# Down products of two pairs in alternate steps, a convolution partly on TensorE at the head, and four places for h's square at the end

## The chip, the cores and the metric

The kernel runs on one core of a Trainium2 chip, as one program. The metric is the device time of one execution in microseconds. TensorE is called PE in the profile, VectorE DVE, ScalarE ACT, GpSimd POOL; SP only issues transfers. DMA queues are marked with a q (SPq, POOLq).

## The reference

Three parts follow one another on 8192 rows of 192 features. First a causal convolution of seven taps over the rows, per head of 24 features, with softmax weights. Then two feed-forward layers of width 2048.

```
w = softmax(weight)                                   # 8 heads x 7 taps
x = sum_k w[head, k] * x_padded[row + k, feature]     # 2 sequences of 4096 rows
h = x @ w_in ;  g = h / (1 + exp(-1.702 h)) ;  x = g @ w_out          # layer 1
h = x @ w_in2 ; P = a0 + a1 h + a2 h^2 + a3 h^3
Q = 1 + |b0| |h| + |b1| h^2 ;  g = P / (Q + 1e-6) ;  out = g @ w_out2 # layer 2
```

## The kernel before

**Tiles and steps.** The rows are worked in 16 tiles (`TILES`) of 512 (`NT`), with features on the partitions. The 192 features are a part a of 128 and a part b of 64. The 2048 columns of a layer are 16 units of 128, taken two at a time: such a pair of units of one tile is a duo in the code, a pair in this text. There are 8 per tile (`DUOS`) and 128 in all (`TOTAL`). The program of each engine is a loop over steps n = 8 i + s. In step n TensorE makes h of layer 1's pair n (`up`, `up_rest`), the down products of layer 1's pair n - 1, h of layer 2's pair n - 10 (`LAG_UP2`) and the down products of layer 2's pair n - 12 (`LAG_DOWN2`). Steps 0 to 9 have layer 1 alone, steps 128 to 139 layer 2 alone (`alone(n)`). Every engine has its own stream in program order; all order between engines is by semaphores that the code writes out by hand. A wait on one engine holds all that stands behind it there.

**Precision.** Each layer's up product is split in high and low parts (`x_a_hi`, `x_a_lo`, `up_a_lo`) in fp32r: eight products of 128 rows per pair and layer (lines `L329` to `L332`), and two of 64 rows (`L356`, `up_rest`), the latter of the two layers side by side on different row halves. Layer 1's 128 output columns are made from parts in fp32r too, six products per pair (`down_a_parts`, `L375` to `L377`), from `g_nhi` and `g_low`. The remaining down products are plain fp32, which the trace shows as two matmuls each: layer 2's 128 columns (`down_a`, `L362`) and both layers' 64 columns (`down_b`, `L382`; for the first tile `down_b_apart`, `L388`). Layer 1's 64 columns go to rows 64 to 127 of the bank `acc_b`, layer 2's to rows 0 to 63.

**The other engines in a step.** ScalarE: for layer 2 `t1` (`L598`), the square of h (`L609`, into `sq`, two places), its absolute value (`L611`); then layer 1's gelu (`L615`, into L1.g, two places) and its rounded negative (`L617`); then for the pair before in layer 2 `s1` and `s2` (`L638`, `L639`) and the reciprocal's seed (`L644`). VectorE: `t2`, `t3`, `q` (`L808`, `L810`, `L811`), `z2` and g (`L832`, `L836`), `z1` (`L846`), and operations of the next tile's convolution (`conv_ops`, `L739`, `L740`), placed by `CONV_AT` and, for tile 1, by `CONV_AT_FIRST`. The reciprocal's product m is GpSimd's (`L961`). From pair 10 on `g_low` comes by two transfers: SP copies g, and POOL's queue adds `g_nhi` to it (`L967`); for the first ten pairs VectorE makes it (`L849`).

**Between the layers.** At s = 0 (`S_X2`) of the next tile ScalarE (`x_a_hi`, `L625`) and VectorE (`L800` to `L802`, `L839`) read layer 1's sums as layer 2's x. At s = 3 (`S_ACC2`) ScalarE copies layer 2's sums into `y_b` and `y_a`; at s = 0 and 1 of the tile after, TensorE turns them and ScalarE writes `y_out`.

**The head.** TensorE turns tile 0 of x, VectorE convolves parts a and b (14 taps), ScalarE rounds the result and the weights' high parts, VectorE makes low parts. Five products with the unit matrix (`L533`) stand before the first step; they have no use in the result.

## Time and profile before

| what | value |
|---|---|
| median of 3 runs | 1317.26 us (1317.21 to 1319.43) |
| the profiled execution | 1320.08 us |
| its span on the core | 1318.3 us |
| TensorE busy, matmuls | 5072 |
| VectorE, ScalarE, GpSimd busy | 1126.2, 1093.1, 533.4 us |
| DMA moved | 148.60 MB, mean 113 GB/s |

The profile is of one execution; the span is what its engines cover, and the execution's time has some 2 us around it. A matmul's end in the records is modelled, so consecutive starts tell more than durations. The idle time before an instruction is printed in brackets with what ended it.

### The profile page before, as it was taken

The numbers are of one execution on the slowest core, as the hardware profiler recorded it, in microseconds if no ns is written. First come the engines' busy times: TensorE is split into PE (matmuls) and PEld (weight loads), VectorE is DVE, ScalarE is ACT, GpSimd is POOL, SyncE is SP. The second block draws the span as 40 slices with busy tenths as digits, with TensorE's granted clock in tenths as the row PEclk, the third lists the DMA queues.
The fourth block names the chain that finished last, engine by engine and source line by source line (L and its number), as shares of the span: only waits on it lengthen the run. The fifth ranks groups of instructions, "written<-read, shape, count | busy, mean of one in ns | idle before, by whom it ended". The sixth has DMA issues, their size and how long they took to land. (4 is left out here: it accounts for less than half of the span.)

```text
span 1318.3 us, 15217 instructions
## 1 busy us (share of the span) xinstructions
PE 1279.1 (97%) x5072; PEld 747.0 (57%) x5072; DVE 1126.2 (85%) x1233; ACT 1093.1 (83%) x1250; POOL 533.4 (40%) x383
## 2 busy tenths in 40 slices
PE   6999999999999999999999999999999999999786
PEld 3556556565665656556565665655556565565432
DVE  6668998989888898988989898898989889777886
ACT  6568898888888888888888888888888888888674
POOL 2414444344443444444444443444434444444221
PEclk9999999999999999999999999999999999999898
DMA  7234445545455554544545454454544555454000
GB/s 183 85 76 114 114 113 132 124 120 136 110 125 117 129 126 115 136 110 124 124 122 134 107 140 113 124 124 109 139 113 124 123 125 116 108 131 105 13 0 24
DMA packets 107822, 148.60 MB, mean 113 GB/s; under 512 B 20961, under 2 KB 45281, under 8 KB 107745
## 3 DMA queue, kind: packets, MB, share of 16 engines
q0 software_dynamic: 33984, 61.88, 27.5%
q1 hardware_dynamic: 73284, 85.75, 19.4%
q8 instruction: 40, 0.66, 0.2%
q14 instruction: 37, 0.30, 0.1%
q10 hardware_dynamic: 477, 0.01, 0.0%
HBM read 13.64 MB, written 6.29 MB: 15 GB/s over the span
## 5 line engine op out<-in xcount | busy, mean ns | idle before, releaser
L961 POOL TENSOR_TENSOR work<-work 128x1024 f32<-128x1024 f32 x127 | 305.1, 2402 | 538.2 <-ACT work L611 491.2
L967 POOL DMA_DIRECT2D g_low<-g_nhi x236 | 207.8, 1015 | 189.8 <-DMA g_low<-g 183.5
L382 PE MATMUL acc_b<-g,down 128*64 128x512 f32 x512 | 248.7, 608 | 11.5 <-DVE g L836 11.4
L362 PE MATMUL acc_a<-g,down 128*128 128x512 f32 x512 | 255.1, 621 | 0.0
L808 DVE TENSOR_TENSOR work<-work,h 128x1024 f32<-128x1024 f32 x128 | 156.3, 1221 | 112.3 <-ACT work L611 110.8
L382 PE MATMUL acc_b<-g,down_b 128*64 128x512 f32 x480 | 231.7, 605 | 0.0
L598 ACT ACTIVATE work<-h,par 128x1024 f32<-128x1024 f32 x128 | 142.5, 1113 | 97.7 <-PE h L356 93.2
L329 PE MATMUL h<-x_a_hi,up_a_hi 128*128 128x512 f32 x510 | 206.8, 406 | 11.1 <-DVE x_a_lo L839 5.5
L331 PE MATMUL h<-x_a_hi,up_a_lo 128*128 128x512 f32 x510 | 199.9, 392 | 0.0
L330 PE MATMUL h<-x_a_lo,up_a_hi 128*128 128x512 f32 x510 | 199.9, 392 | 0.0
L332 PE MATMUL h<-x_b,up_b_hi 128*128 128x512 f32 x510 | 199.6, 391 | 0.0
L638 ACT ACTIVATE work<-work 128x1024 f32<-128x1024 f32 x127 | 134.8, 1062 | 68.0 <-POOL work L961 68.0
L362 PEld LDWEIGHTS acc_a<-g,down 128*128 128x128 f32 x512 | 87.4, 190 | 166.4 <-issue 166.4
L810 DVE SCALAR_TENSOR_TENSOR work<-work,par,h 128x1024 f32<-128x1024 f32 x128 | 164.0, 1281 | 4.5
L811 DVE SCALAR_TENSOR_TENSOR work<-work 128x1024 f32<-128x1024 f32 x128 | 156.2, 1220 | 0.0
L836 DVE SCALAR_TENSOR_TENSOR g<-work 128x1024 f32<-128x1024 f32 x117 | 143.4, 1226 | 11.0 <-issue 0.5
L375 PE MATMUL acc_a<-g_nhi,down_nhi 128*128 128x512 f32 x256 | 150.0, 586 | 2.4 <-DVE g_low L849 1.7
L846 DVE SCALAR_TENSOR_TENSOR work<-work,par 128x1024 f32<-128x1024 f32 x117 | 149.7, 1279 | 1.1 <-ACT work L644 1.1
L615 ACT ACTIVATE g<-h 128x1024 f32<-128x1024 f32 x128 | 132.5, 1035 | 12.8 <-PE h L356 12.8
L832 DVE SCALAR_TENSOR_TENSOR work<-work 128x1024 f32<-128x1024 f32 x117 | 142.7, 1220 | 0.0
L617 ACT ACTIVATE g_nhi<-g 128x1024 fp32r<-128x1024 f32 x128 | 135.9, 1062 | 4.0
L382 PEld LDWEIGHTS acc_b<-g,down 128*64 128x64 f32 x512 | 59.8, 136 | 133.2 <-issue 119.5
(131 smaller groups left out, 1946.7 us busy)
## 6 DMA issues: line engine op xcount, KB each, us to landing
g_low<-g SPq DMA_DIRECT2D x236, 256.0 KB, 2.4
g_low<-g_nhi POOLq DMA_DIRECT2D x236, 256.0 KB, 3.8
out<-y_out SPq DMA_DIRECT2D x15, 384.0 KB, 3.0
x_in<-in_x SPq DMA_DIRECT2D x16, 256.0 KB, 3.1
x_in<-in_x SPq DMA_DIRECT2D x32, 64.0 KB, 2.7
work<-in_moe_w_in SPq DMA_DIRECT2D x8, 256.0 KB, 4.4
work<-in_moe_w_in SPq DMA_DIRECT2D x16, 128.0 KB, 4.6
x_b<-x_hb SPq DMA_DIRECT2D x30, 64.0 KB, 2.1
```

The source lines that it names most:

```text
L329: mm(h, l.up_a_hi[:, cols], l.x_a_hi[:, p, :], start=True, stop=False)
L330: mm(h, l.up_a_hi[:, cols], l.x_a_lo[:, p, :], start=False, stop=False)
L331: mm(h, l.up_a_lo[:, cols], l.x_a_hi[:, p, :], start=False, stop=False)
L332: mm(h, l.up_b_hi[:, cols], l.x_b[:, p, :], start=False, stop=False)
L362: done = mm(L2.acc_a[:], L2.down[:, f, 0:P], L2.g[:, slot, k, :], start=f == 0, stop=f == STEPS - 1)
L375: mm(acc, down_nhi[:, f, :], g_nhi[:, slot, k, :], start=f == 0, stop=False)
L382: return mm(acc_b[l.acc_row:l.acc_row + DB, :], l.down_b[:, f, :], l.g[:, slot, k, :], start=f == 0, stop=f == STEPS - 1)
L808: tt(tu, tu, h, ALU.mult).then_inc(t2_ready, 1)
L810: stt(tu, tu, par[:, 1:2], h, ALU.add, ALU.mult).then_inc(t3_ready, 1)
L811: stt(sk, ab, 1.0 + 1e-6, sk, ALU.add, ALU.add).then_inc(q_ready, 1)
L961: tt(m, sq[v % 2], seed, ALU.mult).then_inc(m_ready, 1)
L967: pool.dma_start(g_low[:, n % 2, k, :], g_nhi[:, n % 2, k, :], accum_op=ALU.add)\
```

## The change

Four things change.

1. **Down products.** Before, every step has the 64-column products of both layers and layer 2's 128-column ones. Now even steps have the 64-column products of two pairs (layer 1's n - 2 and n - 1, layer 2's n - 14 and n - 13), odd steps layer 2's 128-column products of two pairs (n - 13 and n - 12). Layer 1's products from parts stay in every step. `downs` becomes `downs_b` and `downs_a`, with lists `downs1_b`, `downs2_b`, `downs2_a`. The use of g is counted apart for the two kinds (`g1_b_used`, `g2_a_used`, `g2_b_used`), L2.g has three places, and gelu waits for both counts. `S_ACC2` moves from 3 to 4. VectorE's x2 copies move behind `z1`.
2. **The head.** Twelve products of the unit matrix with itself stand ahead of the transposes. ScalarE makes seven diagonal matrices of tap weights, and TensorE convolves part b of tile 0 with them into the bank `first_b`; VectorE does part a alone. Three fillers stay, each behind a tap (`WARM_AFTER`). x_b is rounded before x_a. Tile 1 of x is loaded and turned one step earlier, its convolution spread otherwise, the root's rounds move into steps 0 and 1, and layer 2's weights are made in steps 4 to 7.
3. **The last steps.** `sq_of` gives the square of h two more places, those of L1.g, from pair 122 on (pairs with k % 4 of 2 or 3), so that the square waits for g of four pairs back.
4. **The turn to the end.** In step 128 layer 2's second up product comes after the down products, and x2's low parts are made right behind `q`.

```diff
-S_XT_FIRST = (2, 3)
+S_XT_FIRST = (1, 2)
-S_ACC2 = 3
+S_ACC2 = 4
+S_ACC2_ALONE = 3
-S_WEIGHTS2 = (2, 3, 4, 5)
+S_WEIGHTS2 = (4, 5, 6, 7)
-WARM_AFTER = 9
+WARM_AFTER = (12, 14, 16)
-    CONV_AT_FIRST = (0, 0, 0, 3, 10, NX, NX, NX, NX)
+    CONV_AT_FIRST = (0, 0, 0, 9, 13, NX, NX, NX, NX)
...
+        L2.g = sb("g2", [P, 3, 2, NT])
...
+        def sq_of(k):
+            return L1.g[:, k % 2, :, :] if k + LAG_UP2 >= TOTAL + 2 and k % 4 >= 2 else sq[k % 2]
...
+        def downs2_a(n):
+            if n >= TOTAL + 2:
+                pairs = [n - LAG_DOWN2]
+            else:
+                pairs = [n - LAG_DOWN2 - 1, n - LAG_DOWN2] if n % 2 else []
+            return [v for v in pairs if live(v)]
+        def downs2_b(n):
+            if n == TOTAL + 2:
+                pairs = [n - LAG_DOWN2 - 2, n - LAG_DOWN2 - 1, n - LAG_DOWN2]
+            elif n > TOTAL + 2:
+                pairs = [n - LAG_DOWN2]
+            else:
+                pairs = [n - LAG_DOWN2 - 2, n - LAG_DOWN2 - 1] if n % 2 == 0 else []
+            return [v for v in pairs if live(v)]
+        def downs1_b(n):
+            return [v for v in (n - LAG_DOWN1 - 1, n - LAG_DOWN1) if live(v) and n % 2 == 0]
...
+                    for k in range(2):
+                        if live(v2):
+                            if last(v2):
+                                pe.wait_ge(last_g2, k + 1)
+                            done2 = down_b(L2, e2, v2 % 3, k)
+                        if live(v1):
+                            unit = down_b_apart if v1 < DUOS else down_b
+                            done1 = unit(L1, e1, v1 % 2, k)
...
-                if alone(n):
-                    if n == TOTAL:
-                        up_alone(n)
+                if n == TOTAL:
+                    up_alone(n)
+                elif alone(n):
                     up_alone(n + 1)
-                downs(i, s, v1, v2)
+                downs_b(n)
+                downs_a(n)
+                if n == TOTAL:
+                    up_alone(n + 1)
...
+            for _ in range(12):
+                mm(L1.acc_a[:, 0:P], ident[:], ident[:], start=True, stop=True)
             transpose_x(0, 0)
             transpose_x(0, 1)
             pe.wait_ge(x_evacuated, 2)
-            pe.wait_ge(conv_steps, WARM_AFTER)
-            for _ in range(5):
+            pe.wait_ge(conv_steps, 1)
+            for k in range(taps):
+                pe.wait_ge(diagonal_ready, k + 1)
+                done = mm(L2.h[:, 0, 0:HALF], diagonal[:, k, :], xt_b[:, k:k + HALF], start=k == 0, stop=k == taps - 1)
+            done.then_inc(first_b_done, 1)
+            for count in WARM_AFTER:
+                pe.wait_ge(conv_steps, count)
                 mm(L1.acc_a[:], ident[:], xt_a[:, HALO:], start=True, stop=True)
...
                     wait(act, g1_used, n - 1)
+                    wait(act, g1_b_used, n - 1)
                     fn(L1.g[:, n % 2, :, :], L1.h[:], ACT.Gelu_apprx_sigmoid).then_inc(g1_ready, 1)
```

TensorE, a steady step before, from its last 64-row product on:

```order
L356 MATMUL h2<-x_b2,up_b_lo 128x512
L382 MATMUL acc_b<-g2,down2 64x512 [waits g2_ready,g1_ready]
L382 MATMUL acc_b<-g1,down_b1 64x512
L382 MATMUL acc_b<-g2,down2 64x512
L382 MATMUL acc_b<-g1,down_b1 64x512
L362 MATMUL acc_a2<-g2,down2 128x512 x2
L375 MATMUL acc_a1<-g_nhi,down_nhi 128x512 [waits g1_low_0]
L376 MATMUL acc_a1<-g_nhi,down_nlo 128x512
L377 MATMUL acc_a1<-g_low,down_hi 128x512
```

TensorE now, an even step at the same place (down1's 64 columns are `down_b1`, `L415` is `down_b`, `L408` is `down_a_parts`):

```order
L389 MATMUL h2<-x_b2,up_b_lo 128x512
L415 MATMUL acc_b<-g2,down2 64x512 [waits g2_ready,g1_ready,x2_lo_done]
L415 MATMUL acc_b<-g1,down_b1 64x512
L415 MATMUL acc_b<-g2,down2 64x512
L415 MATMUL acc_b<-g1,down_b1 64x512
L415 MATMUL acc_b<-g2,down2 64x512 [waits g2_ready,g1_ready]
L415 MATMUL acc_b<-g1,down_b1 64x512
L415 MATMUL acc_b<-g2,down2 64x512
L415 MATMUL acc_b<-g1,down_b1 64x512
L408 MATMUL acc_a1<-g_nhi,down_nhi 128x512 [waits g1_low_2]
L409 MATMUL acc_a1<-g_nhi,down_nlo 128x512
```

TensorE now, an odd step at the same place (`L395` is `down_a`):

```order
L389 MATMUL h2<-x_b2,up_b_lo 128x512
L395 MATMUL acc_a2<-g2,down2 128x512 [waits g2_ready]
L395 MATMUL acc_a2<-g2,down2 128x512
L395 MATMUL acc_a2<-g2,down2 128x512 [waits g2_ready]
L395 MATMUL acc_a2<-g2,down2 128x512
L408 MATMUL acc_a1<-g_nhi,down_nhi 128x512 [waits g1_low_0,x2_lo_done,x2_hi_done]
L409 MATMUL acc_a1<-g_nhi,down_nlo 128x512
```

The 64-column products of two pairs stand together in the even step, layer 2's 128-column products of two pairs in the odd one.

ScalarE at the end, the copy into `y_a` and the next pair's operations, before and then now:

```order
L655 ACTIVATE y_a<-acc_a2 128x512 [waits g2_used]
L609 ACTIVATE work<-h2 128x1024 [waits g2_ready]
L611 ACTIVATE work<-h2 128x1024 [waits q_ready]
L598 ACTIVATE work<-h1,par 128x1024 [waits z1_ready,h2_ready]
L638 ACTIVATE work<-work 128x1024 [waits z2_ready,m_ready]
L639 ACTIVATE work<-work 128x1024
L644 ACTIVATE work<-work 128x1024 [waits m_ready,z1_ready,q_ready]
```

```order
L734 ACTIVATE y_a<-acc_a2 128x512 [waits g2_a_used]
L680 ACTIVATE g1<-h2 128x1024 [waits g2_ready]
L682 ACTIVATE work<-h2 128x1024 [waits q_ready]
L662 ACTIVATE work<-h1,par 128x1024 [waits z1_ready,h2_ready]
L710 ACTIVATE work<-work 128x1024 [waits z2_ready,m_ready]
L711 ACTIVATE work<-work 128x1024
L716 ACTIVATE work<-g1 128x1024 [waits m_ready,z1_ready,q_ready]
```

The square (`L609` before, `L680` now) goes into g1 instead of work, and the seed (`L644`, `L716`) reads it there.

## Rows read from the trace of the kernel before

**Rows 1.** The page, part 1: busy time, share of the span, instructions.
```profile
PE 1279.1 (97%) x5072; PEld 747.0 (57%) x5072; DVE 1126.2 (85%) x1233; ACT 1093.1 (83%) x1250; POOL 533.4 (40%) x383
```

**Rows 2.** Waits of TensorE, 130 to 1210 us: total, times, longest.
```profile
PE acc_b L382 <- DVE g L836: 0.7, 3, 0.3
```

**Rows 3.** Timeline of TensorE, one steady step: start us, us, engine, line, operation.
```profile
613.27 0.39 PE L329 MATMUL h<-x_a_hi,up_a_hi 128*128 128x512 f32 x1
...
616.67 0.39 PE L332 MATMUL h<-x_b,up_b_hi 128*128 128x512 f32 x1
...
616.99 0.73 PE L356 MATMUL h<-x_b,up_b_lo 64*128 64x512 f32 x4
...
618.56 0.59 PE L382 MATMUL acc_b<-g,down 128*64 128x512 f32 x1
...
618.99 0.59 PE L382 MATMUL acc_b<-g,down 128*64 128x512 f32 x1
...
619.52 1.99 PE L362 MATMUL acc_a<-g,down 128*128 128x512 f32 x4
...
621.57 0.39 PE L376 MATMUL acc_a<-g_nhi,down_nlo 128*128 128x512 f32 x1
...
622.72 0.39 PE L329 MATMUL h<-x_a_hi,up_a_hi 128*128 128x512 f32 x1
```

**Rows 4.** Timeline of all engines, around a gelu of the steady stretch.
```profile
1195.96 0.64 PE L382 MATMUL acc_b<-g,down 128*64 128x512 f32 x1
...
1198.92 1.04 ACT L615 ACTIVATE g<-h 128x1024 f32<-128x1024 f32 x1
...
1200.40 1.28 DVE L810 SCALAR_TENSOR_TENSOR work<-work,par,h 128x1024 f32<-128x1024 f32 x1
...
1202.85 0.39 PE L329 MATMUL h<-x_a_hi,up_a_hi 128*128 128x512 f32 x1
```

**Rows 5.** Timeline of TensorE and VectorE, steps 1 to 14.
```profile
22.44 0.48 PE L329 MATMUL h<-x_a_hi,up_a_hi 128*128 128x512 f32 x1 [1.20 <-ACT g L615]
...
45.54 0.39 PE L332 MATMUL h<-x_b,up_b_hi 128*128 128x512 f32 x1
...
47.86 0.40 PE L376 MATMUL acc_a<-g_nhi,down_nlo 128*128 128x512 f32 x1
...
48.04 1.79 DVE L740 SCALAR_TENSOR_TENSOR conv_a<-xt_a,wts,conv_a 128x512 f32<-128x512 f32 x1
...
54.78 0.77 PE L375 MATMUL acc_a<-g_nhi,down_nhi 128*128 128x512 f32 x1 [1.65 <-DVE g_low L849]
...
74.20 0.39 PE L329 MATMUL h<-x_a_hi,up_a_hi 128*128 128x512 f32 x1
...
111.59 0.48 PE L329 MATMUL h<-x_a_hi,up_a_hi 128*128 128x512 f32 x1
```

**Rows 6.** Timeline of TensorE, VectorE and ScalarE, before the first step.
```profile
4.63 1.09 PE L395 MATMUL turned<-ident,x_in 128*128 128x128 f32 x4 [4.63 <-DMA x_in<-in_x]
...
11.19 7.56 PE L533 MATMUL acc_a<-xt_a,ident 128*128 128x512 f32 x10 [5.05 <-DVE conv_b L740]
...
14.14 0.75 DVE L740 SCALAR_TENSOR_TENSOR conv_a<-xt_a,wts,conv_a 128x512 f32<-128x512 f32 x1
...
15.20 0.75 DVE L740 SCALAR_TENSOR_TENSOR conv_a<-xt_a,wts,conv_a 128x512 f32<-128x512 f32 x1
...
15.98 0.63 ACT L563 ACTIVATE x_a_hi<-conv_a 128x512 fp32r<-128x512 f32 x1 [0.33 <-DVE conv_a L740]
...
18.19 1.03 PE L340 MATMUL h<-x_a_hi,up_a_hi 128*128 128x512 f32 x2
```

**Rows 7.** The end: timeline of TensorE, then VectorE's waits (1250 to 1300, 1232 to 1300).
```profile
1227.69 0.77 PE L329 MATMUL h<-x_a_hi,up_a_hi 128*128 128x512 f32 x1 [5.53 <-DVE x_a_lo L839]
...
DVE work L808 <- ACT work L611: 4.0, 6, 0.8
...
DVE x_in L832 <- ACT work L638: 2.0, 1, 2.0
```

More of the change, by code:

```diff
@@ new lines, in downs_a @@
+            def downs_a(n):
+                v1 = n - LAG_DOWN1
+                for v2 in downs2_a(n):
+                    if v2 == 0:
+                        pe.wait_ge(down2_loaded, 16 * CHUNKS)
+                    if v2 % DUOS == 0:
+                        wait(pe, acc2_a_read, v2 // DUOS)
+                    if last(v2):
+                        pe.wait_ge(last_g2, 2)
+                    else:
+                        pe.wait_ge(g2_ready, v2 + 1)
+                    down_a(v2).then_inc(g2_a_used, 1)
@@ L686, in _ @@
             evacuate_x(0, 0)
+            act.wait_ge(setup_dve, 6)
+            for k in range(taps):
+                fn(diagonal[:, k, :], ident[:], ACT.Copy, scale=wts[:, 1, k:k + 1]).then_inc(diagonal_ready, 1)
             weights_hi(L1, 0, stage1, w1_hi)
@@ L743, in keep, with first, first_end @@
                     return ts(dst, src, 1.0, None, ALU.mult)
+                def first():
+                    front().then_inc(conv_steps, 1)
+                    keep(halo_a[:, at], xt_a[:, NT:NT + HALO]).then_inc(conv_steps, 1)
+                    keep(halo_b[:, at], xt_b[DB:P, HALF:HALF + HALO]).then_inc(conv_steps, 1)
+                    tap(0, 0).then_inc(conv_steps, 2)
+                    clear(halo_a).then_inc(conv_steps, 1)
+                    clear(halo_b).then_inc(conv_steps, 1)
+                    for k in range(1, taps):
+                        dve.wait_ge(conv_steps, 2 * k + 5)
+                        tap(k, 0).then_inc(conv_steps, 2)
+                def first_end():
+                    dve.wait_ge(first_b_done, 1)
+                    dve.wait_ge(conv_steps, CONVOLVED)
+                    keep(xt_a[:, 0:HALO], halo_a[:, at]).then_inc(conv_steps, 1)
+                    keep(xt_b[0:DB, 0:HALO], halo_b[:, at]).then_inc(conv_steps, 1)
                 def clear(halo):
@@ L756, in conv_ops @@
                 assert len(ops) == NX
+                if tile == 0:
+                    return first, first_end
                 def ordered(op, done):
@@ L784, in down_lo, with x2_a_lo, x2_b @@
                     ALU.mult, ALU.subtract).then_inc(d1_nlo, 1)
+            def x2_a_lo(t, p):
+                dve.wait_ge(x2_hi_done, t + 1)
+                tt(L2.x_a_lo[:, 1 - p, :], L1.acc_a[:], L2.x_a_hi[:, 1 - p, :].bitcast(F32), ALU.subtract)\
+                    .then_inc(x2_lo_done, 1)
+            def x2_b(t, p):
+                dve.wait_ge(g1_b_used, DUOS * (t + 1))
+                wait(dve, h2_ready, DUOS * (t - 1))
+                whole = acc_b
+                if t == 0:
+                    whole = x2_part
+                    nc.vector.tensor_copy(x2_part[DB:P, :], acc_b[0:DB, :]).then_inc(x2_part_read, 1)
+                    dve.wait_ge(x2_part_read, 1)
+                    tt(x2_part[DB:P, :], acc_b[DB:P, :], x2_part[DB:P, :], ALU.add).then_inc(x2_part_added, 1)
+                    dve.wait_ge(x2_part_added, 1)
+                nc.vector.tensor_copy(L2.x_b[DB:P, 1 - p, :], whole[DB:P, :]).then_inc(x2_b_hi_done, 1)
+                dve.wait_ge(x2_b_hi_done, t + 1)
+                tt(L2.x_b[0:DB, 1 - p, :], whole[DB:P, :], L2.x_b[DB:P, 1 - p, :].bitcast(F32), ALU.subtract)\
+                    .then_inc(x2_lo_done, 1)
             def step(i, s, p, conv, at):
@@ L834, in step @@
                     dve.wait_ge(z2_ready, v + 1)
-                    wait(dve, g2_used, v - 1)
+                    wait(dve, g2_a_used, v - 2)
+                    wait(dve, g2_b_used, v - 2)
                     stt(gv, s2, d2, zv, ALU.add, ALU.mult).then_inc(g2_ready, 1)
-                if s == S_X2 and tile_live(t):
-                    dve.wait_ge(x2_hi_done, t + 1)
-                    tt(L2.x_a_lo[:, 1 - p, :], L1.acc_a[:], L2.x_a_hi[:, 1 - p, :].bitcast(F32), ALU.subtract)\
-                        .then_inc(x2_lo_done, 1)
+                if n < LAG_UP2:
+                    dve.wait_ge(g1_nhi_ready, n + 1)
+                    tt(g_low[:, n % 2, :, :], L1.g[:, n % 2, :, :], g_nhi[:, n % 2, :, :].bitcast(F32), ALU.add)\
+                        .then_inc(g1_low_first, 1)
+                    if n < CHUNKS:
+                        down_lo(n)
+                if s == S_X2 and tile_live(t) and not alone(n):
+                    x2_a_lo(t, p)
                 if live(u):
@@ L905, in chunk0_b_lo @@
                     .then_inc(w1_lo_first, 1)
[L907 to L909 removed]
+            first, first_end = conv_ops(0)
+            first()
             dve.wait_ge(w1_hi, 1)
```

199 lines of the change are left out of this document (97 added, 102 removed).

## The prediction

> **What bounds the kernel now.** I read the totals first. TensorE (PE) is busy for 97% of the span, VectorE (DVE) for 85% and ScalarE (ACT) for 83% [rows 1]. The list of waits for 130 to 1210 us comes next: its longest entry for TensorE is 0.7 us in 1080 [rows 2]. So in the steady stretch nothing feeds TensorE too late, and the time is what its own stream takes. The timeline of one steady step shows that stream [rows 3]: a step runs from the `L329` at 613.27 to the one at 622.72, 9.45 us, with no idle time. Consecutive 128-row fp32r products start 0.23 us apart, and the two halves of a plain fp32 product 0.43 us apart (618.56, 618.99), whether 64 or 128 columns wide; two 64-column products on different halves of the output rows go side by side in one such slot.
>
> Inside that step is time that no product fills. The last `L332` starts at 616.67 and is through at 616.90. The first `L375` begins 0.23 before the `L376` at 621.57, so at 621.34 (a record's start can lie in the matmul before it, so I take the next one's start less one spacing). Between lie 4.44 us. The 64-row products fill two slots of 0.23, the 64-column ones four of 0.43, the 128-column ones four of 0.43: 3.90. The other 0.54 lies at three places where the shape of the tile changes: 128 x 128 to 64 rows, 64 rows to 64 columns, 64 columns back to 128. The last of these can be read alone: the 64-column products end at 618.99 + 0.43 = 619.42, the 128-column ones must have begun at 621.34 - 1.72 = 619.62, so it costs **0.20**. From plain fp32 `L362` to fp32r `L375`, same shape, nothing is lost.
>
> At both ends the kernel is not bound by TensorE's stream. At the head TensorE first waits for x and for the convolution, then steps 1 to 9 have one layer only, with a stall. In the last twelve steps layer 2 runs alone in a chain through VectorE.
>
> **The steady stretch.** Before, two steps have six changes of shape. Now an even step has three (64 rows, 64 columns, 128) and an odd one two (64 rows, 128), and the number of products is the same. That removes one change per two steps. Steps 14 to 127 are 57 such pairs: 57 x 0.20 = **-11.4 us**. The new step from 64 rows straight to plain fp32 of 128 columns is shown by no row. Its ends are 0 and twice the 0.20; the nearest rows are the three changes, 0.54 / 3 = 0.18 on average, and I take it equal to the one it replaces. The head has the same average where 64-column products are followed directly by `L375`: from 45.54 + 0.23 to 47.86 - 0.23 are 1.86 us, less two slots of 0.23 and two of 0.43 leaves 0.54 again for three changes [rows 5]. The Trainium skill, TensorEngine Tiling (Array Packing), Key Properties, says that changing the tiling mode drains TensorE, while changing only the tile does not; it gives no price. By that rule the saving is one drain per two steps and the sum is the same; a cost that hung on the number format instead would save nothing, and that is a rival below.
>
> The waits that this adds must stay hidden. An even step's gelu (`L615` before) now also needs the 64-column products of the pair two steps back, which stand first in the same step. They begin at 1195.96 and take four slots, 1.72, so they release it near 1197.7, while that gelu starts at 1198.92 because three ScalarE operations of layer 2 stand before it [rows 4]: 1.2 us of cover. The gelu ends at 1199.96 and layer 1's next up products start at 1202.85 - 8 x 0.23 = 1201.01: 1.05 to spare. `t3` (`L810`) ends at 1201.68 against 1202.85: 1.17 to spare. After an odd step TensorE arrives 0.20 sooner, which both bear. The third place of g2 lets layer 2's pair be used one step later; VectorE's wait for the 64-column product of three pairs back is released at the same early point. The x2 copies of VectorE move behind `z1`, but layer 1's 64-column sum starts again only two steps after it ended, so TensorE has a step more. The accumulating transfers of g_low must be there 0.20 sooner in odd steps; I put 0.3 of risk there, within the rounding of the sum. ScalarE's copies out of layer 2's sums move one step later together with the sums.
>
> **The head.** Twelve unit-matrix products of 128 columns now stand ahead of the transposes. At the slow level (1.2 GHz) half a 512-column fp32 product takes about 0.85 us (`L533`, ten records in 7.56 us) [rows 6], so 24 halves of a quarter of that take 5.1 us. Only two short GpSimd operations precede them; starting near 1.5 (an estimate) they end at 6.6. Before, the transposes start at 4.63. They end some 2 us later now, but VectorE read them only after the softmax chain, so the convolution starts about 0.9 us later, not 2. It then has seven taps rather than fourteen on VectorE: instead of one a-tap per 1.06 us (14.14 to 15.20, a b-tap between) one of 0.75 that waits for the one before, 0.78. So six taps gain 6 x 0.28 = 1.7 and the a-part ends near 15.2 instead of 15.95 [rows 6]. The b-part is seven products on TensorE, 0.43 us each at 2.4 GHz and 0.85 at 1.2 GHz, 3 to 6 us from about 10. ScalarE makes seven diagonal matrices first (an estimate, 2 us), then its weights, then x_b and x_a. I get x_a near 16.9, where before TensorE had it at 15.98 + 0.63 = 16.6 but was held to 18.19 by its own filler products [rows 6]. The three fillers now end near 17.6. The first h is ready about 1 us earlier: **-1.0**, with ends -2 (all at the fast level) and +2 (the transposes' delay is passed on whole).
>
> **Steps 1 to 9** took 74.20 - 22.44 = 51.8 us [rows 5]. The stream now: five odd steps without 64-column products, 8 x 0.23 + 2 x 0.23 + 6 x 0.23 + 2 x 0.18 = 4.04; four even ones with two pairs of them, four slots, 4.04 + 4 x 0.43 + 0.20 = 5.96. Together 44.0. Four rounds of transposes come to about 1.4 (the four of 4.63 took 1.09 at the slow level, some 0.5 here; an estimate): 45.4. What can be lost on top is a stall like the one before: at 54.78 TensorE had stood 1.65 us for `g_low`, behind VectorE's convolution of tile 1, and after that standstill the clock was at the lower level for seven products and more, 0.43 in place of 0.23, about 1.3 us. That convolution now starts a step earlier (9 operations in step 2, 4 in step 3, 8 in step 4) and x is loaded and turned earlier for it. I allow 0.9 of loss: 46.3, so **-5.5**, ends -6.4 and -2.
>
> **Steps 10 to 13** took 111.59 - 74.20 = 37.4. Once layer 2 runs, gelu ends 1199.96 - 1195.96 = 4.0 us after the down products begin [rows 4]; with few down products that chain sets steps 10 and 11, before and after. Step 12 loses layer 2's four 128-column slots (1.72), since those of pair 0 now come in step 13 in place of the 64-column ones, and the change of shape between: **-2.0**, ends -0.5 and -2.5.
>
> **The end.** Here each pair's `L808` waits for the absolute value `L611`, which stands behind the square, which waited for g of two pairs back: 4.0 us in six waits [rows 7]. With two more places the square of pairs 122 to 127 waits for g of four pairs back. Each wait of 0.67 shrinks to a hand-over of under 0.1, and VectorE's own six operations then set the pace. That gives 6 x 0.6 = 3.6. Against it: y copies of tile 14 (one of 512 columns, which took 0.63 in the row at 15.98 [rows 6], and two narrower, 1.3 in all) now stand together right before pair 122's square, and y_out copies stand twice before later squares, where the slack is gone: +1.9. In step 128 layer 1's last products now come before the second half of up products, so x2 is ready some 4 us sooner than the 1227.6 that released TensorE after 5.53 idle us [rows 7], and VectorE does t2, t3, q before it waits for acc_b. VectorE stood 2.0 us for ScalarE on that account (`L832` [rows 7]), and I add 0.9 for t2 (ends 0 and 2.0): 2.9. Together 3.6 + 2.9 - 1.9 = **-4.6**, ends -2 and -6.5.
>
> **Sum:** -11.4 - 1.0 - 5.5 - 2.0 - 4.6 = -24.5. The profiled execution took 1320.08 (span 1318.3), so 1295.6 against it. The median of the three runs is 2.8 lower, 1317.26, and I predict **1292.8**.
>
> **The rivals.**
> *The stall stays* (0.14). VectorE's taps slow down beside GpSimd's weight halves: one took 1.79 instead of 0.75 at 48.04, where GpSimd worked on `up_b_lo` [rows 5]. Layer 2's weights are now made in steps 4 to 7 instead of 2 to 5, just where eight convolution operations of step 4 stand. If two or three taps are held so, g_low comes late again, TensorE stands and the clock falls: 3 us back at the stall and 2 in the steps after, 1298. The Trainium skill, SBUF — State Buffer, Who interferes with whom, says of this that VectorE operations with two SBUF inputs and GpSimd operations lock each other out for a whole instruction; the row at 48.04 agrees, since that tap took about 1 us more.
> *Format, not shape* (0.08). If what costs is the entry into plain fp32 together with a narrow tile, the odd step pays 0.40 at its new change: nothing from the steady stretch, 1304.
> *The end gives nothing* (0.07). POOL's product (2.4 us) and three ScalarE operations stand in the same loop; if they set it, the pace of a pair stays: 1297.
> *Slower* (0.03). One mechanism: the even step's gelu is released late. It decides once the release comes over 1.2 + 1.05 = 2.25 us later than above, that is near the end of the step's down products; beyond it each us costs one us in 59 even steps. It needs 2.7 us of delay to eat 24.5 us; at 3 us it gives 1337. For it speaks only that one engine now waits within a step; against it, that the release is on the first pair's own products.
> *Nothing changes beyond 0.2%* (0.02).
>
> **How the numbers follow.** Full forecast 0.66, its own range 1288 to 1298. The first three rivals are faster too: faster 0.95, same 0.02, slower 0.03. Within 0.2% (2.6 us) this kernel can't be told from unchanged. All ends added would give 1285 to 1305; the range is 1287.5 to 1302, which leaves out the unlucky end of the format rival.
>
> **What would show it.** Starts of up products 9.45 us apart after even and 9.25 after odd steps; no wait of TensorE over 0.5 us between 130 and 1200. No TensorE idle time near 50 us and steps 1 to 9 in 46. First gelu about 1 us earlier. No wait of `L808`'s counterpart for the absolute value over 0.1 in the last pairs. Steps of 9.45 throughout would show the shape theory wrong; a gelu that waits for the 64-column products would show the last rival at work.

## The result, and the profile after

The changed kernel takes **1299.7 us** (median of 4 runs, 1299.32 to 1300.63), the kernel before beside it 1318.14 us (4 runs): a ratio of **0.986** with a 95% interval of 0.984 to 0.988. The profiled execution took 1299.79 us with a span of 1298.0, against 1320.08 and 1318.3. The forecast was 1292.8 with a range of 1287.5 to 1302.0: the range holds the result, the full forecast's own 1288 to 1298 does not.

The page's first part, of after (busy time, share, instructions; compare [rows 1], where TensorE is busy 1279.1 us; the 5072 of the table is its matmuls):

```profile
PE 1271.7 (98%) x5106; PEld 755.3 (58%) x5106; DVE 1119.5 (86%) x1226; ACT 1094.4 (84%) x1257; POOL 531.9 (41%) x383
```

The timeline of TensorE, of after, one even step (from 600.91) and one odd step (from 610.39), with the columns of [rows 3]. `L362` to `L365` are now the up products, `L389` the 64-row ones, `L415` the 64-column ones, `L395` layer 2's of 128 columns, `L408` to `L410` those from parts:

```profile
600.91 0.40 PE L362 MATMUL h<-x_a_hi,up_a_hi 128*128 128x512 f32 x1
...
604.65 0.73 PE L389 MATMUL h<-x_b,up_b_lo 64*128 64x512 f32 x4
605.31 0.64 PE L415 MATMUL acc_b<-g,down 128*64 128x512 f32 x1
...
608.37 0.59 PE L415 MATMUL acc_b<-g,down_b 128*64 128x512 f32 x1
608.89 0.50 PE L408 MATMUL acc_a<-g_nhi,down_nhi 128*128 128x512 f32 x1
...
610.39 0.39 PE L362 MATMUL h<-x_a_hi,up_a_hi 128*128 128x512 f32 x1
...
614.11 0.73 PE L389 MATMUL h<-x_b,up_b_lo 64*128 64x512 f32 x4
614.77 3.70 PE L395 MATMUL acc_a<-g,down 128*128 128x512 f32 x8
617.91 0.79 PE L408 MATMUL acc_a<-g_nhi,down_nhi 128*128 128x512 f32 x1
...
619.69 0.40 PE L362 MATMUL h<-x_a_hi,up_a_hi 128*128 128x512 f32 x1
```

The even step is 9.48 us long, 0.03 more than a step before, and the odd one 9.30; two together are 18.78 where before they were 2 x 9.45 [rows 3]. From the last 128-row product to the first product from parts an even step has 0.54 us that no product fills (three changes of shape), an odd one, by the same reckoning, 0.39 (two): the change that is gone was worth 0.15.

The starts of the single matmuls in both traces give each change its own price. Two starts lie further apart than inside a run (0.23 us for fp32r and for 64 rows, 0.43 for plain fp32). Before, into 64 rows: 616.67, 616.99, 617.33, together 0.66 for 0.46, so 0.20. Into 64 columns: 617.33, 617.65, 618.13, so 0.14. Back to 128 columns: 618.99, 619.52, 620.05, so 0.20. And in the odd step of after, from 64 rows straight into 128 columns: 614.45, 614.77, 615.30, so 0.19.

TensorE waits for nothing between 130 and 1190 us.

Stages by the starts of the up products, from the timelines of both (steps are counted from 0; of before the starts are those of [rows 5] and 1211.19 for step 128, of after the bounds of the next fence):

| stretch | before | after | difference | forecast |
|---|---|---|---|---|
| start to step 1 | 22.44 | 20.53 | -1.9 | -1.0 |
| steps 1 to 9 | 51.76 | 45.48 | -6.3 | -5.5 |
| steps 10 to 13 | 37.39 | 37.24 | -0.15 | -2.0 |
| steps 14 to 127 | 1099.60 | 1090.58 | -9.0 | -11.4 |
| step 128 to the end of the span | 107.11 | 104.17 | -2.9 | -4.6 |
| sum | 1318.3 | 1298.0 | -20.3 | -24.5 |

The same stretches, of after, as busy times (x instructions) of each engine, with TensorE's granted clock, the share of DMA and GB/s at the end:

```profile
20.53:66.01 45.48, 45.13 (x184) 28.37 (x185) 30.29 (x50) 32.32 (x46) 16.87 (x13) 1.00 0.39 107
66.01:103.25 37.24, 35.19 (x133) 21.01 (x132) 30.40 (x41) 27.07 (x28) 11.78 (x9) 1.00 0.40 95
103.25:1193.83 1090.58, 1090.11 (x4491) 657.19 (x4489) 963.20 (x1029) 953.82 (x1076) 475.65 (x343) 1.00 0.52 123
1193.83:1298.00 104.17, 86.45 (x239) 38.17 (x239) 84.95 (x76) 68.61 (x83) 25.48 (x12) 0.95 0.07 20
```

Only the last stretch has much time in which TensorE stands, and a clock under 1.00. Its timeline of TensorE, of after:

```profile
1265.62 1.93 PE L415 MATMUL acc_b<-g,down 128*64 128x512 f32 x4 [1.01 <-DVE g L947]
...
1273.42 2.47 PE L415 MATMUL acc_b<-g,down 128*64 128x512 f32 x4 [3.63 <-DVE g L947]
1275.82 3.10 PE L395 MATMUL acc_a<-g,down 128*128 128x512 f32 x4
1281.17 3.38 PE L415 MATMUL acc_b<-g,down 128*64 128x512 f32 x4 [2.26 <-DVE g L947]
1284.49 2.18 PE L395 MATMUL acc_a<-g,down 128*128 128x512 f32 x4
1286.51 2.74 PE L580 MATMUL acc_a<-xt_a,ident 128*128 128x512 f32 x6
1289.17 1.93 PE L415 MATMUL acc_b<-g,down 128*64 128x512 f32 x4
```

Here the last gate of VectorE (g of the last pair, `L938`; the gates are the input of the down products) ends at 1285.19 + 1.28 = 1286.47, but its products start at 1289.17. TensorE has stood 3.63 and 2.26 us for gates, the products behind these waits take up to 3.4 us instead of 1.93, and then three filler products (`L580`, six records; their result is never used) still stand in front. The kernel before has the same three fillers in the same place (`L525`). Of before, the fillers, the last gate and the last products:

```profile
1306.72 2.74 PE L525 MATMUL acc_a<-xt_a,ident 128*128 128x512 f32 x6
1307.05 1.29 DVE L828 SCALAR_TENSOR_TENSOR g<-work,x_in 128x512 f32<-128x512 f32 x2
1309.39 1.93 PE L382 MATMUL acc_b<-g,down 128*64 128x512 f32 x4
```

There the gate ends at 1308.34, and TensorE was still at its fillers then. The granted clock in these places, of after (stretches of 4 us, columns as above):

```profile
1274.00:1278.00 4.00, 4.00 (x7) 1.32 (x6) 3.77 (x4) 1.47 (x2) 2.36 (x1) 0.58 0.29 98
1281.00:1285.00 4.00, 3.83 (x5) 1.14 (x6) 3.63 (x6) 1.76 (x4) 0.00 (x0) 0.57 0.00 0
```

Most of either stretch is at the lower of the clock's two levels, 1.2 GHz in place of 2.4. The fillers themselves ran at the upper one: from 1285 to 1290 the granted clock is 1.00. That pointed at the fillers' place, and at the clock.

### The profile page after: what moved, and what is told of

It reads as the page before. It is cut to its first block, busy times and chain, and to the rows that moved or that the text cites. A ratio compares the mean times of both kernels' runs of the same rounds, so it can differ in the third digit from the quotient of the medians.

```text
span 1298.0 us, 15435 instructions
## 1 busy us (share of the span) xinstructions
PE 1271.7 (98%) x5106; PEld 755.3 (58%) x5106; DVE 1119.5 (86%) x1226; ACT 1094.4 (84%) x1257; POOL 531.9 (41%) x383
## 3 DMA queue, kind: packets, MB, share of 16 engines
q1 hardware_dynamic: 73284, 85.75, 19.7%
## 4 chain that ended last, share of the span: by engine, by line
PE 91%; DVE 3%; ACT 3%; issue 1%; POOL 1%; DMA 0%; SPq 0%; DVEq 0%; POOLq 0%; ACTq 0%
PE acc_b L415 17%; PE acc_a L395 16%; PE h L362 9%; PE h L364 9%; PE h L363 9%; PE h L365 9%; PE h L389 7%; PE acc_a L408 6%; PE acc_a L410 5%; PE acc_a L409 4%; POOL work L1072 1%; DVE g L947 1%; DVE x_in L942 1%; PE acc_b L421 1%; ACT work L682 1%
## 5 line engine op out<-in xcount | busy, mean ns | idle before, releaser
L1072 POOL TENSOR_TENSOR work<-work 128x1024 f32<-128x1024 f32 x124 | 298.0, 2403 | 501.8 <-ACT work L682 433.4
L914 DVE TENSOR_TENSOR work<-work,h 128x1024 f32<-128x1024 f32 x128 | 156.2, 1220 | 119.1 <-ACT work L682 118.8
L415 PE MATMUL acc_b<-g,down 128*64 128x512 f32 x512 | 236.2, 603 | 10.7 <-DVE g L947 10.7
L395 PE MATMUL acc_a<-g,down 128*128 128x512 f32 x512 | 239.5, 609 | 0.0
L415 PE MATMUL acc_b<-g,down_b 128*64 128x512 f32 x480 | 218.8, 598 | 0.0
L362 PE MATMUL h<-x_a_hi,up_a_hi 128*128 128x512 f32 x510 | 205.8, 404 | 4.4 <-issue 1.6
L365 PE MATMUL h<-x_b,up_b_hi 128*128 128x512 f32 x510 | 199.2, 391 | 0.0
L395 PEld LDWEIGHTS acc_a<-g,down 128*128 128x128 f32 x512 | 92.3, 191 | 120.9 <-issue 106.4
L917 DVE SCALAR_TENSOR_TENSOR work<-work 128x1024 f32<-128x1024 f32 x124 | 151.3, 1221 | 0.0
L415 PEld LDWEIGHTS acc_b<-g,down 128*64 128x64 f32 x512 | 64.7, 137 | 144.6 <-issue 130.6
L942 DVE SCALAR_TENSOR_TENSOR work<-work 128x1024 f32<-128x1024 f32 x117 | 142.6, 1219 | 0.2
L408 PE MATMUL acc_a<-g_nhi,down_nhi 128*128 128x512 f32 x256 | 131.8, 515 | 2.0 <-DMA g_low<-g_nhi 1.5
```

Source lines behind the costliest of these rows:

```text
L362: mm(h, l.up_a_hi[:, cols], l.x_a_hi[:, p, :], start=True, stop=False)
L365: mm(h, l.up_b_hi[:, cols], l.x_b[:, p, :], start=False, stop=False)
L395: done = mm(L2.acc_a[:], L2.down[:, f, 0:P], L2.g[:, v % 3, k, :], start=f == 0, stop=f == STEPS - 1)
L408: mm(acc, down_nhi[:, f, :], g_nhi[:, slot, k, :], start=f == 0, stop=False)
L415: return mm(acc_b[l.acc_row:l.acc_row + DB, :], l.down_b[:, f, :], l.g[:, slot, k, :], start=f == 0, stop=f == STEPS - 1)
L914: tt(tu, tu, h, ALU.mult).then_inc(t2_ready, 1)
```

## The experiments

All stand beside runs of the kernel before. The changed kernel, repeated as a yardstick:

> The changed kernel once more, as the common yardstick of the runs beside it: 1299.7 us, and 0.986 of the kernel before.

Measured 1299.69 us (1299.19 to 1300.17), ratio 0.9862 [0.9846, 0.9879]; once more in the second set, `after_tail`:

> The changed kernel again, as the yardstick of the three runs beside it: 1299.7 us.

1300.07 us (1298.74 to 1302.08), 0.9856 [0.9842, 0.9869]. Their traces give a measure of chance. Steps 14 to 127 took 1090.58, 1090.50 and 1091.68 us, the longest with three waits of TensorE for the transfer of `g_low` that the first does not have (1.0 us in all). The steps 10 to 13 took 37.24, 38.34 and 37.14. The stretch from step 128 took 104.17, 102.5 and 102.5 us: the first has the low clock behind both gate waits, the others behind one. The last gate ends 92.6 us after the start of step 128 in all three, where before it was 97.15.

The head has two forms. In these three traces and that of no_end_fill the twelve warm products took 4.4 to 4.6 us, TensorE's convolution 3.26 and VectorE's first tap stands at 9.1. In the six others that have these products (shape_split, format_split, each_step, old_spread, old_sq, early_fill) they took 5.05 to 5.49, the convolution 4.95, and the first tap stands at 9.40 to 10.14. Layer 1's first product starts at 16.3 to 16.4 in the first form and at 16.6 to 17.3 in the second, 18.19 before. No edit touches the products of the head in any of the ten; what decides is open.

### Shape or format: shape_split, format_split

```diff
+            def mixed(n):
+                return 16 <= n < 124 and n % 2 == 0
...
                             done1 = unit(L1, e1, v1 % 2, k)
+                        if mixed(n) and at == 1 and k == 0:
+                            down_a_parts(n - LAG_DOWN1, (n - LAG_DOWN1) % 2, (0,))
...
-                    down_a_parts(v1, v1 % 2).then_inc(g1_used, 1)
+                    down_a_parts(v1, v1 % 2, (1,) if mixed(n) else (0, 1)).then_inc(g1_used, 1)
```

> In the 54 even steps from 16 to 122 the second pair's 64-column down products are issued in two halves with half of the 128-column products of layer 1's parts between them: the same products, two more changes of tile shape in each even step. Theory 'a change of shape has a price': one change into 64 columns (about 0.15 us) and one into 128 columns (0.195 us), 0.34 us a step, so +18 us over the changed kernel (1318 us), and the first product of each run follows the one before it later than its neighbours do. Rival 'the price hangs on the hand-over between layer 1 and layer 2 or on a wait for the gates': nothing is added, 1300 us. Rival 'the price hangs on the number format' expects the same +18 us here, since the halves also alternate between plain and reduced fp32; format_split tells it from the first.

Measured **1317.94 us** (10 runs, 1317.31 to 1320.48), 0.9997 [0.9987, 1.0006]: 18.25 us over the changed kernel beside it, or 0.338 per step for two changes (by the trace steps 14 to 127 take 1110.26 us, 19.7 more). The whole gain of the change is gone, with the same products. The timeline of TensorE and of its weight loads (PEld) shows both seams, of shape_split:

```profile
637.23 0.40 PE L409 MATMUL acc_a<-g_nhi,down_nlo 128*128 128x512 f32 x1
637.46 0.40 PE L410 MATMUL acc_a<-g_low,down_hi 128*128 128x512 f32 x1
637.79 0.64 PE L415 MATMUL acc_b<-g,down 128*64 128x512 f32 x1
...
638.27 0.59 PE L415 MATMUL acc_b<-g,down 128*64 128x512 f32 x1
...
638.80 0.50 PE L408 MATMUL acc_a<-g_nhi,down_nhi 128*128 128x512 f32 x1
639.13 0.39 PE L409 MATMUL acc_a<-g_nhi,down_nlo 128*128 128x512 f32 x1
```
```profile
637.23 0.19 PEld L410 LDWEIGHTS acc_a<-g_low,down_hi 128*128 128x128 f32 x1
637.79 0.13 PEld L415 LDWEIGHTS acc_b<-g,down 128*64 128x64 f32 x1 [0.37 <-issue]
...
637.84 0.14 PEld L415 LDWEIGHTS acc_b<-g,down 128*64 128x64 f32 x1
...
638.79 0.19 PEld L408 LDWEIGHTS acc_a<-g_nhi,down_nhi 128*128 128x128 f32 x1 [0.81 <-issue]
638.90 0.19 PEld L409 LDWEIGHTS acc_a<-g_nhi,down_nlo 128*128 128x128 f32 x1
```

Inside a run the load of the next weights stands one product ahead (0.23 us in fp32r, 0.43 in plain fp32): `L410`'s at 637.23, its product at 637.46. At a seam it does not: `L415`'s load and product both have 637.79, `L408`'s 638.79 and 638.80. Into 64 columns the starts are 0.33 and 0.48 apart, where inside a run they are 0.23 and 0.43: 0.15 lost. Into 128 columns 0.53 and 0.33 stand for 0.43 and 0.23: 0.20 lost. The loads take 0.13 and 0.19. So what a change costs here is about the weight load that no longer lies beside a product. A fixed price of 0.17 for each would fit the medians as well; that the two seams differ as their loads do speaks for the load, and no run changed the load alone.

The Trainium skill, TensorEngine Tiling (Array Packing), Key Properties, says that changing the tiling mode drains TensorE. The seams agree in that each costs time, 0.15 and 0.20 us, and format_split below in that a change without another shape costs none.

```diff
+            def mixed(n):
+                return 16 <= n < 124 and n % 2 == 1
...
+                    if mixed(n):
+                        down_a_parts(v1, v1 % 2, (0,))
+                        down_a(n - LAG_DOWN2, (1,)).then_inc(g2_a_used, 1)
+                        down_a_parts(v1, v1 % 2, (1,)).then_inc(g1_used, 1)
```

> In the 54 odd steps from 17 to 123 layer 2's plain-fp32 products of 128 columns and layer 1's reduced-fp32 products of 128 columns are issued in halves by turns: two more changes of number format in each odd step, and not one more of tile shape. Theory 'the shape has the price': +0, 1299 to 1301 us, and no gap at the seams. Rival 'the format has the price': two more changes of 0.16 to 0.20 us in 54 steps, +17 to +22 us, 1317 to 1321 us.

Measured **1299.26 us** (4 runs), 0.9865 [0.9848, 0.9881]: nothing. The odd step's down products, of format_split:

```profile
633.89 2.84 PE L395 MATMUL acc_a<-g,down 128*128 128x512 f32 x6
...
637.26 1.02 PE L395 MATMUL acc_a<-g,down 128*128 128x512 f32 x2
...
638.81 0.60 PE L428 MATMUL turned<-ident,x_in 128*128 128x128 f32 x4
```

From 633.89 to 638.81 are 4.92 us, with four changes of format; after has 614.77 to 619.69, also 4.92, with two. The rival "format, not shape" falls.

### The order of the down products alone: each_step

The order goes back, and with it `S_ACC2`, the place of the x2 copies and the waits that hang on them (not shown); L2.g keeps its third place.

```diff
         def downs2_a(n):
-            if n >= TOTAL + 2:
-                pairs = [n - LAG_DOWN2]
-            else:
-                pairs = [n - LAG_DOWN2 - 1, n - LAG_DOWN2] if n % 2 else []
-            return [v for v in pairs if live(v)]
+            return [v for v in (n - LAG_DOWN2,) if live(v)]
...
-            return [v for v in (n - LAG_DOWN1 - 1, n - LAG_DOWN1) if live(v) and n % 2 == 0]
+            return [v for v in (n - LAG_DOWN1,) if live(v)]
```

> Down products of one pair in every step as before the change, the head and the end as after it. Theory: the steps from 14 to 127 go back to 9.45 us each, +0.158 us in each of 57 pairs of steps, so +9 us, and the steps 10 to 13, where the grouped order gained only 0.15 us, lose about nothing: 1308 to 1310 us. Rival 'the grouping is worth the 11.4 us of the forecast and something else in the changed kernel costs 2.4 us': 1311 us or more. Rival 'the head and the end bring the most': under 1304 us.

Measured **1310.6 us** (4 runs), 0.9947 [0.993, 0.9963]. By its trace steps 14 to 127 take 1098.41 us, 7.8 more than after (0.137 for a pair of steps; 9 was expected), steps 10 to 13 take 37.36 (+0.1, as expected), and steps 1 to 9 take 47.60 (+2.1), which I had not expected: there too the grouping takes a change of shape out of two steps. The head was 0.7 later (its second form). The end was 0.7 shorter than in the profiled after and 0.9 longer than in the two repeats, where the last gate comes 0.9 sooner. The median lies between the theory's 1308 to 1310 and the 1311 of the first rival; the stretches speak for the theory, and the rival "the head and the end bring the most" falls. So the order of the down products is worth some 10 of the 18 us (10.9 by the medians); the head and the end give the rest.

### The stall at the head: old_spread

```diff
-S_XT_FIRST = (1, 2)
+S_XT_FIRST = (2, 3)
-S_WEIGHTS2 = (4, 5, 6, 7)
+S_WEIGHTS2 = (2, 3, 4, 5)
-    CONV_AT_FIRST = (0, 0, 0, 9, 13, NX, NX, NX, NX)
+    CONV_AT_FIRST = (0, 0, 0, 3, 10, NX, NX, NX, NX)
```

> The spread of the first tile's tables is as before the change: layer 1's x for the second tile is transposed in steps 2 and 3, VectorE's first convolution units come from step 3 on, and layer 2's weights are requested in steps 2 to 5; all else as in the changed kernel. With the order of the down products as before (each_step), steps 1 to 10 took 47.6 us in place of the changed kernel's 45.48 us; the kernel before took 51.76 us. Theory 'this spread is what took the stall near 50 us away': the stall returns and the steps 1 to 10 take 3 to 4 us more, +3 to +4 us at the end, 1303 to 1304 us. Rival 'the convolution of the head on TensorE took it away, VectorE being early enough now': within 0.5 us of 1299.8 us.

Measured **1302.37 us** (4 runs), 0.9875 [0.986, 0.989]: 2.3 to 2.7 us over the changed kernel in the two other sets, under the +3 to +4 expected. Steps 1 to 9 take 48.43 us (21.52 to 69.95), 2.95 more. The waits of TensorE between 16 and 70 us, of old_spread (in all, times, longest):

```profile
PE acc_a L408 <- DVE g_low L950: 2.2, 3, 1.5
PE h L362 <- ACT g L687: 1.2, 1, 1.2
```

After has no wait for `g_low` in these steps. The stall of [rows 5] came back with the old spread although TensorE does part of the convolution at the head: the spread took it away, and the rival falls. The edit puts three things back at once (the turning, the convolution's places, layer 2's weights); which of them counts is not told apart. With the grouping's 2.1 it makes 5.1 of the 6.3 us.

### The end: old_sq, no_end_fill

The wait in front of the square goes back with its place (not shown).

```diff
-            return L1.g[:, k % 2, :, :] if k + LAG_UP2 >= TOTAL + 2 and k % 4 >= 2 else sq[k % 2]
+            return sq[k % 2]
```

> The square of h keeps its two places at the end too. Theory of the forecast: the last gates wait for a place again, which was forecast to be worth 4.6 us with the order of the end; step 128's start to the second gelu of pair 127 measured 4.5 us less after the change, the whole end 2.9 us less. So +2.3 to +3.6 us, 1302 to 1303.3 us, and GpSimd's or VectorE's wait for a place (2.0 us on the gate's row before the change) is back in the last four pairs. Rival 'the end's gain is that of the down products' order alone': within 0.5 us of the changed kernel.

Measured **1301.89 us** (4 runs), 0.9871 [0.9856, 0.9886]: +1.8 us, under the range. VectorE's waits from 1215 us on, of old_sq (`L907` is the first of its six operations on a pair):

```profile
DVE work L907 <- ACT work L675: 5.6, 8, 1.1
```

and of after:

```profile
DVE work L914 <- ACT work L682: 2.8, 5, 1.0
```

The wait is where the forecast said (0.65 us per pair, pairs 8.2 us apart; after has 7.7). By the traces the stretch from step 128 is 104.9 us, 2.4 over the two yardsticks with the same number of low-clock runs. The last gate ends 95.0 us after the start of step 128, against 92.6 with the four places and 97.15 before: of the 4.5 us that this chain got shorter, 2.4 are the places' and 2.2 that of all else in the end (the turn and the order), which was not run alone.

```diff
                 if last(n - LAG_DOWN2 + 1):
-                    for _ in range(3):
-                        mm(L1.acc_a[:], ident[:], xt_a[:, HALO:], start=True, stop=True)
+                    pass
```

> The three filler products in front of the last down products are left out (their result is never used). In the changed kernel's profile they start at 1286.51 us, when the last gate is just ready (1286.48 us), and take 2.7 us at a low clock, and the last down products start at 1289.17 us. Theory 'the fillers stand in the way since the last gate comes earlier': -1.5 to -2.7 us, 1297 to 1298.2 us. Rival 'they buy the clock of the last products and of the way out': the products behind them take longer, 0 to +2 us.

Measured **1297.40 us** (5 runs), 0.9835 [0.9822, 0.9849]: -2.7 us. The last products kept their speed, of no_end_fill:

```profile
1280.94 3.21 PE L415 MATMUL acc_b<-g,down 128*64 128x512 f32 x4 [3.91 <-DVE g L946]
1284.08 2.36 PE L395 MATMUL acc_a<-g,down 128*128 128x512 f32 x4
1286.36 1.93 PE L415 MATMUL acc_b<-g,down 128*64 128x512 f32 x4
```

The rival that the fillers buy the clock of the last products finds nothing here. The trace does not bear all of the 2.7 out: its end is 101.6 us, 0.9 under the yardstick's, and the rest lies in the steps before, which the edit does not touch.

### The warming products of the head, and both together: no_first12, lean

```diff
-            for _ in range(12):
-                mm(L1.acc_a[:, 0:P], ident[:], ident[:], start=True, stop=True)
```

> The first 12 products with the unit matrix at the head are left out (their result is never used). Theory 'they raise the granted clock while the inputs load and nothing waits for them': the first transposes run at the low clock and the first up product starts up to 1 us later, +0 to +1 us. Rival 'TensorE is late itself there': the first step starts earlier, -0.3 to -1 us. Rival 'the loads end last': within 0.2 us of the changed kernel.

Measured **1297.65 us** (5 runs), 0.9834 [0.9821, 0.9848]: -2.4 us, which neither theory had. At the head, with cold transposes and a slower convolution (5.75 us in place of 3.26), the first up products start at 16.61 instead of 16.31, as the first theory said. But kernels with the twelve products in the head's second form start them as late or later (16.6 to 17.3), so no gain of theirs is shown. The 2.4 us are not at the end either (102.5 us, the same). The largest part that the traces show is in steps 14 to 127 (1090.1 against 1091.7), where the code is the same.

The direction comes back in the pairs below: lean against no_end_fill -1.05 us, early_fill_lean against early_fill -1.2, both across sets. In the three traces without the twelve, steps 14 to 127 take 1090.11, 1089.76 and 1089.54 us, in the seven with the twelve and the same code in these steps 1090.36 to 1091.68. So it is more than the chance of one pair, but what causes it stays open.

> Both kinds of filler products are out: the 12 with the unit matrix at the head and the three in front of the last down products. Singly they gave 1297.65 us and 1297.40 us beside 1300.07 us. Theory 'the two gains are apart': 1295 us. Rival 'both are one gain, that of where the low clock falls at the end': 1297 to 1298 us.

Measured **1296.35 us** (5 runs), 0.9832 [0.9818, 0.9845]: between the two. TensorE's last products, of lean:

```profile
1272.91 3.06 PE L415 MATMUL acc_b<-g,down 128*64 128x512 f32 x4 [3.64 <-DVE g L944]
...
1280.66 1.93 PE L415 MATMUL acc_b<-g,down 128*64 128x512 f32 x4 [2.26 <-DVE g L944]
...
1285.41 1.93 PE L415 MATMUL acc_b<-g,down 128*64 128x512 f32 x4 [0.91 <-DVE g L935]
```

The low clock falls in the same place as in `after_tail`, so the two ends compare: 100.9 against 102.5 us. That is the fillers' cost, **1.6 us**, and TensorE now waits 0.91 for the last gate: VectorE's chain sets the end. From the end of the last gate to the end of the span are 8.3 us here, 9.9 in the two repeats and 9.95 in the kernel before. So the fillers seem to cost the kernel before as much as the changed one; no run took them out of it.

### Fillers in the gaps: early_fill, early_fill_lean

```diff
+                if last(n - LAG_DOWN2 + 2) or last(n - LAG_DOWN2 + 1):
+                    for _ in range(3):
+                        mm(L1.acc_a[:], ident[:], xt_a[:, HALO:], start=True, stop=True)
                 downs_b(n)
                 downs_a(n)
```

> The three fillers in front of the last down products are out, and three stand instead in front of the down products of each of the two pairs before the last but one and the last but one, where TensorE waits 3.63 and 2.26 to 3.9 us for a gate. Theory 'TensorE's idle time in the tail brings the low clock, and the last down products wait for the slow ones before them': the granted clock stays high from 1270 us on, each run of four 64-column products takes 1.93 us, the last run starts with the first half of the last gate, -0.4 to -1 us against the kernel with no fillers at the end (1297.4 us), so 1296.4 to 1297 us. Rival 'the low clock hides behind the gates': 1297.4 us.

Measured **1297.27 us** (5 runs), 0.9837 [0.9824, 0.9851]. The fillers fit into the gaps, the granted clock is 1.00 in both of the stretches shown for after, and the last products wait for the gate, of early_fill:

```profile
1270.35 2.74 PE L574 MATMUL acc_a<-xt_a,ident 128*128 128x512 f32 x6
1274.14 1.93 PE L415 MATMUL acc_b<-g,down 128*64 128x512 f32 x4 [1.05 <-DVE g L949]
...
1281.88 1.93 PE L415 MATMUL acc_b<-g,down 128*64 128x512 f32 x4 [1.32 <-DVE g L949]
...
1286.63 1.93 PE L415 MATMUL acc_b<-g,down 128*64 128x512 f32 x4 [0.91 <-DVE g L940]
```

Its end is 100.9 us, as in lean, against 101.6 in no_end_fill, where the low clock fell on the products just before the last; the medians (1297.27 and 1297.40) do not tell the two apart. So the early fillers only remove that case.

> early_fill without the 12 products with the unit matrix at the head. In the trace of early_fill the stretch from the third-last step's up products to the end is 0.66 us shorter than in no_end_fill, as expected, but the medians are alike (1297.27 and 1297.40 us), and in lean's trace the low clock falls on the products at 1273 us, where a gate hides it. Theory 'the early fillers only make sure of what lean has by where its low clock falls': the same as lean, 1296.0 to 1296.5 us. Rival 'they are worth 0.66 us on top': 1295.7 us.

Measured **1296.05 us** (5 runs, 1295.77 to 1297.25), 0.9828 [0.9815, 0.9842], the fastest version, though not told apart from lean. Both beat the kernel before and the changed one.

## Why the forecast held, and where its sum was off

The direction was right, and so was the mechanism of every term but that of steps 10 to 13. The sum was 6.9 us too low. Of these, 4.2 are in the terms (24.5 against 20.3). The other 2.7 are the step from the profiled execution to the median: I took 2.8 off because the profiled execution of before was that much above its median; after's was only 0.1 above. That median was of three runs; in the later sets the kernel before has 1318.4 to 1318.9.

That the range holds the result is in part luck. Its upper part was there for the rivals, and none of them came true; the forecast's own range missed by 1.7. The sentence on the ends is wrong too: the ends as written add up to 1277 to 1315, or to 1288 to 1303 with the steady stretch held at -11.4, and not to 1285 to 1305.

**The steady stretch** (-11.4, measured -9.0). The step that failed is "57 x 0.20". The new change from 64 rows into 128 columns does cost what the one that it replaces did, 0.19 and 0.20, as I had taken. What is gone is the change into 64 columns, and I priced it by the only seam that I had read alone, the one into 128. It costs 0.14 to 0.15, by its own starts in the trace of before and by shape_split. each_step has 0.137 per pair of steps: 57 x 0.14 to 0.15 is 8.0 to 8.6; the rest of the 9.0 is within what one kernel's traces differ by. The average of 0.18 that I had beside it was nearer. The waits that I had called hidden were hidden: TensorE waits for nothing there. That the shape costs and the format does not, is shown by the pair of runs.

**Steps 10 to 13** (-2.0 with ends -0.5 and -2.5, measured -0.15; with the repeats -0.25 to +0.95). The step that failed is "Step 12 loses layer 2's four 128-column slots". It does, but I kept the 64-column products at four slots. Before, step 12 issues one pair's with layer 2's beside them. Now it issues two pairs of layer 1, and layer 2's pair 0 comes in step 14, so nothing goes beside them. The same in step 10, of after:

```profile
70.39 3.65 PE L415 MATMUL acc_b<-g,down_b 128*64 128x512 f32 x8
```

Eight slots of 0.43. Step 10 gets 1.0 longer (9.46 us, which is its own stream and no longer the chain through gelu), and the slots that step 11 is rid of bring it 0.3, because TensorE then waits for g_low (0.99 and 0.53 us, at 80.91 and 82.39).

**The head** (-1.0, measured -1.9 in the profiled execution). The step that was off is "the convolution starts about 0.9 us later": the warm products ran from 1.53 to 6.08, not to 6.6, the clock was up for the transposes and for the convolution on TensorE (3.26 us), and VectorE's first tap stands at 9.10, where before it was at 9.09. In the head's second form the tap does come 0.3 to 1.1 later, and the first up product starts 0.9 to 1.6 sooner than before. So the forecast has one form and the profiled execution the other.

**Steps 1 to 9** (-5.5, measured -6.3). The stall rival fell: no wait for g_low, and the 45.5 us are the 45.4 that I had counted for the stream alone, so the 0.9 allowed for a loss was not lost. The mechanism of that rival is still there without harm: `L819` took 1.83 us instead of 0.74 at 42.35, where GpSimd worked on `up_a_lo`, but the gates had the slack.

**The end** (-4.6, measured -2.9 in the profiled execution, -4.6 in the two repeats). The chain through VectorE got 4.5 us shorter in all three, as forecast. The parts cancel: 2.4 for the places (1.7 forecast, 3.6 less the copies' 1.9) and 2.2 for the turn and the order (2.9 forecast). The loop's wait shrank as forecast in the last five pairs, from 0.65 to 0.25 and less. What the forecast did not price is TensorE behind that chain. In the profiled execution the low clock fell behind both gate waits; the fillers then start at 1286.51, 92.7 us after the start of step 128 in place of 91.0 in the repeats, and the 1.7 us between -4.6 and -2.9 are lost. The fillers' own 1.6 us are no part of this miss, since the kernel before has them too. The rival "the end gives nothing" fell.

The signs: starts 9.48 and 9.30 us apart (9.45 and 9.25 named); no wait in the steady stretch; no standstill near 50 us and 45.5 us for steps 1 to 9 (46 named); the first gelu at 19.36 in place of 21.28 (about 1 us named); in the last five pairs `L914` waits 0.20 to 0.25 where y_out copies stand before it and not at all in the other three (0.1 named). The rival "slower" did not come true, but its mechanism shows at the head: the gelus at 29.08, 39.06 and 59.80 (steps 2, 4 and 8) waited for the 64-column products of their step, ScalarE standing 0.7, 2.0 and 2.0 us. TensorE did not wait for them. In the steady stretch no gelu waits so.

## What to carry to other kernels

When TensorE is the bound and never waits, count the changes of tile shape in its stream, not only its products: each costs 0.14 to 0.20 us here, and putting like shapes together costs only buffers and order. Price each change by its own seam. Fillers that keep the clock up belong where TensorE waits anyway; in front of the product that everything waits for, they can end later than its input comes, which cost 1.6 us here.

## What was not expected of the hardware

- At a change of tile shape the load of the next weights has the same start as its product; elsewhere it stands one product ahead, 0.23 or 0.43 us. A change of number format within one shape costs nothing (4.92 and 4.92 us).
- After waits of TensorE of 2.3 to 4.0 us the granted clock fell behind some and not behind others at the same place in the program: the four 64-column products behind such a wait took 1.93, 2.47 or up to 3.57 us, so that the end of one and the same kernel was 102.5 or 104.2 us long. Where six filler records stood in the gap, it did not fall.
- The same warm products at the head took 4.4 to 4.6 us in four traces and 5.05 to 5.49 in six, and the first up product started up to 1.0 us later in the second case.
